# Attention in a gated MLP kernel: where the probabilities are divided by their sums

## The reference, cut to what matters

```python
k_sum = k.reshape(B, H, nb, block, D).max(axis=3)
v_sum = v.reshape(B, H, nb, block, D).mean(axis=3)
scores_l = scale * np.matmul(q, k.transpose(0, 1, 3, 2))
mask_l = np.abs(pos[:, None] - pos[None, :]) < window
scores_s = scale * np.einsum('bhsd,bhnd->bhsn', q, k_sum) + np.log(block)
scores_all = np.concatenate([np.where(mask_l, scores_l, -1e9), scores_s], axis=-1)
a = np.exp(scores_all - np.max(scores_all, axis=-1, keepdims=True))
a = a / (np.sum(a, axis=-1, keepdims=True) + 1e-09)
attn_out = np.matmul(a, np.concatenate([v, v_sum], axis=2))
```

## Time and profile before

| | us |
|---|---|
| median of 3 runs | 357.35 |
| lowest and highest | 356.35 and 358.55 |
| span of the profiled execution | 357.2 |
| VectorE busy in the span | 233.7 |
| TensorE busy in the span | 320.7 |
| ScalarE and GpSimd busy in the span | 150.7 and 136.4 |

### The profile page before, as it was taken

One profiled execution on the slowest core, in us unless ns is written; L12 is line 12 of the kernel. 1 busy time (PEld: TensorE's weight loads), 2 busy tenths in 40 slices (PEclk: granted clock), 3 DMA queues, 4 the chain that ended last, 5 costly groups with the idle time before them and its releaser, 6 DMA issues.

```text
span 357.2 us, 5495 instructions
## 1 busy us (share of the span) xinstructions
PE 320.7 (90%) x1876; PEld 292.6 (82%) x1876; DVE 233.7 (65%) x638; ACT 150.7 (42%) x416; POOL 136.4 (38%) x118
## 2 busy tenths in 40 slices
PE   8777967775778899996999999999999999999997
PEld 7666856765668788985799999988889999998886
DVE  6799999999999999979888200028886633331000
ACT  3375656664677676363322322243333211112222
POOL 5219367339434212599205700004444933331000
PEclk9899899999999999999899999999999999999999
DMA  8896774266331221233100000011211000001222
GB/s 180 143 212 146 164 167 108 62 157 143 91 87 50 57 67 59 73 119 89 46 0 1 2 0 2 0 44 46 73 30 31 29 2 0 0 2 59 88 109 98
DMA packets 49721, 25.33 MB, mean 71 GB/s; under 512 B 44170, under 2 KB 44446, under 8 KB 49310
## 3 DMA queue, kind: packets, MB, share of 16 engines
q1 hardware_dynamic: 49694, 24.99, 27.7%
HBM read 21.24 MB, written 3.15 MB: 68 GB/s over the span
## 4 chain that ended last, share of the span: by engine, by line
PE 56%; DVE 23%; issue 10%; POOL 5%; DMA 3%; SPq 1%; ACT 1%; DVEq 0%; POOLq 0%
PE psum L592 52%; DVE probs L858 6%; DVE neg_s L839 6%; DVE gate L901 3%; POOL g_lo L458 2%; DMA v_blk<-in_v_dram 2%; DVE sums_eps L847 2%; POOL win_v_lo L458 2%; DVE k_max L871 1%; DVE recip L852 1%; PE psum L675 1%; DVE k_a L880 1%; POOL win_u_lo L458 1%; PE psum L544 1%; DMA raw<-in_moe_w_in_dram 1%
## 5 line engine op out<-in xcount | busy, mean ns | idle before, releaser
L858 DVE TENSOR_SCALAR probs<-probs,recip 128x184 f32<-128x184 f32 x96 | 60.9, 675 | 1.7
L718 ACT ACTIVATE probs<-neg_s,neg_max 128x184 f32<-128x184 f32 x96 | 42.2, 441 | 44.8 <-DVE neg_max L839 44.5
L458 POOL TENSOR_TENSOR g_lo<-work,g_hi 128x384 fp32r<-128x384 f32 x32 | 36.3, 1147 | 46.8 <-ACT g_hi L819 25.8
L544 PE MATMUL psum<-ident,probs 128*128 128x128 f32 x144 | 25.8, 288 | 22.4 <-DVE probs L858 22.1
L901 DVE SCALAR_TENSOR_TENSOR gate<-xT,conv_c,gate 128x384 f32<-128x384 f32 (+8 forms) x44 | 41.7, 956 | 1.3
L544 PEld LDWEIGHTS psum<-ident,probs 128*128 128x128 f32 x144 | 16.0, 143 | 29.4 <-DVE probs L858 28.7
L458 POOL TENSOR_TENSOR vn_lo<-work,vn_hi 128x512 fp32r<-128x512 f32 x12 | 15.5, 1293 | 57.2 <-DVE vn_hi L1040 57.2
L839 DVE CUSTOM_DVE_ANT_0 neg_s<-psum,mask 128x184 f32<-128x184 f32 x96 | 29.2, 340 | 0.0
L1018 DVE TENSOR_TENSOR wsp_lo<-psum,wsp_hi 128x384 fp32r<-128x384 f32 x12 | 6.6, 548 | 33.6 <-ACT wsp_hi L800 33.6
L458 POOL TENSOR_TENSOR x_lo<-xT,x_hi 128x768 fp32r<-128x768 f32 x8 | 15.0, 1869 | 32.2 <-DVE x_hi L863 32.2
L1050 DVE TENSOR_TENSOR work<-psum,b_row 128x384 f32<-128x384 f32 x16 | 8.9, 558 | 27.8 <-PE psum L592 26.2
(11 more groups left out here) (125 smaller groups left out, 791.3 us busy)
## 6 DMA issues: line engine op xcount, KB each, us to landing
k_nat<-in_k_dram SPq DMA_DIRECT2D x16, 192.0 KB, 3.2
q_nat<-in_q_dram SPq DMA_DIRECT2D x16, 192.0 KB, 3.3
v_blk<-in_v_dram SPq DMA_DIRECT2D x4, 768.0 KB, 7.6
out_dram<-work SPq DMA_DIRECT2D x11, 256.0 KB, 2.0
v_main<-in_v_dram SPq DMA_DIRECT2D x16, 160.0 KB
raw<-in_moe_w_spatial_dram SPq DMA_DIRECT2D x6, 384.0 KB, 3.0
raw<-in_moe_w_out_dram SPq DMA_DIRECT2D x8, 256.0 KB, 2.7
raw<-in_moe_w_in_dram SPq DMA_DIRECT2D x8, 256.0 KB, 2.9
```

Source lines behind the costliest of these rows:

```text
L458: nc.gpsimd.tensor_tensor(dst_lo, src, dst_hi.bitcast(F32), ALU.subtract).then_inc(lo_sem, 1)
L544: ins = nc.tensor.transpose(bank_t(i)[:, n * P:(n + 1) * P], probs[:, i % 4, c:c + P], ident[:, :])
L718: ins = nc.scalar.activation(probs[:, i % 4, w], neg_s[:, i % 3, w], ACT.Exp, bias=neg_max[:, i % 4, h:h + 1], scale=-1.0, accum_out=sums[ ...
L858: ins = nc.vector.tensor_scalar(a, a, recip[:, i % 4, h:h + 1], None, ALU.mult)
```

## The change

The probabilities go into the products undivided. `invert_sums` writes the reciprocal of each of the two sums of a row 64 times, into a tile of 128x128 instead of 128x2. A TensorE transpose with the identity (`spread_recip`) lays this tile over the rows of the transposed output: row d of head h holds, at column q, the reciprocal of the sum of query q in head h. It goes into the two free quarters of the bank that holds the output of the same steps. ScalarE copies the undivided output to `xT` as before, but waits for the transposes, and a new VectorE instruction, `scale_x`, multiplies `xT` in place with the spread reciprocals from PSUM, for two steps at once. `high_x` and the taps wait for `scale_x`. On VectorE `normalise` goes, `scale_x` stands at the start of every odd step, and the loop has four steps more; the last halves of taps and the last two `split_wout` are placed anew in them. The exponentials wait for `add_eps` of four steps before.

```diff
--- before.py
+++ after.py
@@ -120,7 +120,7 @@
                 neg_max = sb("neg_max", [P, 4, 2], F32, att)
                 sums = sb("sums", [P, 4, 2], F32, att)
                 sums_eps = sb("sums_eps", [P, 4, 2], F32, att)
-                recip = sb("recip", [P, 4, 2], F32, att)
+                recip = sb("recip", [P, 4, P], F32, att)
                 probs = sb("probs", [P, 4, SC], F32, att)
                 probsT = sb("probsT", [P, 2, 3 * P], F32, att)
             win_v_hi = sb("win_v_hi", [P, C, DM], F32R, early)
@@ -164,7 +164,8 @@
         exp_done = sem("exp_done")
         eps_added = sem("eps_added")
         recip_ready = sem("recip_ready")
-        probs_ready = sem("probs_ready")
+        spread_done = sem("spread_done")
+        x_taken = sem("x_taken")
         probs_turned = sem("probs_turned")
         probsT_ready = sem("probsT_ready")
         x_summed = sem("x_summed")
@@ -537,7 +538,7 @@
                                  stop=True).then_inc(scores_ready, 1)
 
             def turn_probs(i):
-                pe.wait_ge(probs_ready, i + 1)
+                pe.wait_ge(exp_done, i + 1)
                 if i >= 2:
                     pe.wait_ge(probsT_ready, i - 1)
                 for n, c in enumerate((MAIN_A, MAIN_B, REST)):
@@ -560,6 +561,12 @@
                 nc.tensor.matmul(o, v_main[:, s, t, D:D + P], pT[:, P:2 * P], start=False, stop=False)
                 nc.tensor.matmul(o, v_rest[:, s, t, :], pT[:, 2 * P:3 * P], start=False,
                                  stop=True).then_inc(x_summed, 1)
+
+            def spread_recip(i):
+
+                pe.wait_ge(recip_ready, i + 1)
+                n = 2 * P + i % 2 * P
+                nc.tensor.transpose(bank_x(i)[:, n:n + P], recip[:, i % 4, :], ident[:, :]).then_inc(spread_done, 1)
 
             def turn_wout(c):
                 wait_piece(pe, W_OUT + c)
@@ -645,6 +652,7 @@
                     turn_probs(i - 3)
                 if 4 <= i:
                     values(i - 4)
+                    spread_recip(i - 4)
 
             for kind, n in groups[2:place["u", 0]]:
                 if kind == "val":
@@ -713,6 +721,7 @@
                 act.wait_ge(masked, i + 1)
                 if i >= 4:
                     act.wait_ge(probs_turned, i - 3)
+                    act.wait_ge(eps_added, i - 3)
                 for h in range(2):
                     w = slice(h * HEAD, (h + 1) * HEAD)
                     ins = nc.scalar.activation(probs[:, i % 4, w], neg_s[:, i % 3, w], ACT.Exp,
@@ -733,10 +742,10 @@
 
             def take_x(j):
 
-                act.wait_ge(x_summed, 2 * j + 2)
+                act.wait_ge(spread_done, 2 * j + 2)
                 p, r = divmod(2 * j, T)
                 nc.scalar.activation(xT[:, p, r * P:(r + 2) * P], bank_x(2 * j)[:, 0:2 * P],
-                                     ACT.Copy).then_inc(xT_ready, 1)
+                                     ACT.Copy).then_inc(x_taken, 1)
 
             def turned_wout(c):
                 act.wait_ge(wout_turned, c + 1)
@@ -849,14 +858,18 @@
 
             def invert_sums(i):
                 dve.wait_ge(eps_added, i + 1)
-                nc.vector.reciprocal(recip[:, i % 4, :], sums_eps[:, i % 4, :]).then_inc(recip_ready, 1)
-
-            def normalise(i):
-                dve.wait_ge(recip_ready, i + 1)
-                for h in range(2):
-                    a = probs[:, i % 4, h * HEAD:(h + 1) * HEAD]
-                    ins = nc.vector.tensor_scalar(a, a, recip[:, i % 4, h:h + 1], None, ALU.mult)
-                ins.then_inc(probs_ready, 1)
+                if i >= 4:
+                    dve.wait_ge(spread_done, i - 3)
+                nc.vector.reciprocal(recip[:, i % 4, :].rearrange("p (h d) -> p h d", d=D),
+                                     sums_eps[:, i % 4, :].rearrange("p (h d) -> p h d", d=1).broadcast_to(
+                                         (P, 2, D))).then_inc(recip_ready, 1)
+
+            def scale_x(j):
+
+                dve.wait_ge(x_taken, j + 1)
+                p, r = divmod(2 * j, T)
+                x = xT[:, p, r * P:(r + 2) * P]
+                nc.vector.tensor_tensor(x, x, bank_x(2 * j)[:, 2 * P:4 * P], ALU.mult).then_inc(xT_ready, 1)
 
             def high_x(p):
                 dve.wait_ge(xT_ready, T // 2 * (p + 1))
@@ -945,10 +958,10 @@
                 conv(tap // TAPS, tap % TAPS, (half,))
                 halves_done += 1
 
-            for i in range(STEPS + 2):
+            for i in range(STEPS + 6):
                 p, t = divmod(i, T)
-                if i >= 2:
-                    normalise(i - 2)
+                if i >= 7 and i % 2 == 1:
+                    scale_x((i - 7) // 2)
                 if i == 0:
                     add_blocks(0)
                 if i == 1:
@@ -962,7 +975,7 @@
                     mask_scores(i, 1)
                 if 0 <= i - 1 < STEPS:
                     add_eps(i - 1)
-                if t == 5 and p >= 1:
+                if t == 5 and 1 <= p < PAIRS:
                     high_x(p - 1)
                 if i < STEPS and p >= 2 and (t in (0, 1, 4) or p == PAIRS - 1):
                     conv_half()
@@ -975,11 +988,11 @@
                     split_wout(i - 2 - (PAIRS - 1) * T)
                 if 0 <= i - 1 < STEPS:
                     invert_sums(i - 1)
-                if i >= STEPS:
-                    for _ in range(3):
+                if i in (STEPS + 1, STEPS + 2):
+                    split_wout(i - STEPS + 1)
+                if STEPS <= i < STEPS + 4:
+                    for _ in range(2):
                         conv_half()
-            split_wout(2)
-            split_wout(3)
             while halves_done < 2 * TAPS * ATT_GATES:
                 conv_half()
             high_x(PAIRS - 1)
```

## The result

The changed kernel takes 359.44 us, the median of 20 runs (358.1 to 362.53), against 357.46 of the kernel before (20 runs, 355.57 to 359.85): a ratio of 1.0063, 95% interval 1.0039 to 1.0087. It is 0.6% slower, some 2 us, where 12 us were forecast. The profiled execution has a span of 357.4 us, only 0.2 more than before.

The account below looks back on a forecast made before the run. VectorE was taken to bound attention: work -30.7 + 45.6 + 8.4 = +23.3 us, held time -11.5, waits +2, with some 1.5 hidden, made +12: 369 us. Its own range was 362 to 374, the full range 345 to 377.

Parts of the forecast that it names:

- Part 1: VectorE in attention: two normalisations and the old reciprocal leave 48 steps, 30.7 us less work, held time not counted.
- Part 2: VectorE in attention: the widened reciprocal at 7 ns per element, 0.95 us in each of 48 steps, 45.6 us added.
- R1: Rival, chance 0.30: the reciprocal is short (0.28 us) and a loop through ScalarE's copy and scale_x sets attention, 348 us.
- Part 3: VectorE in attention: scale_x every other step, 24 x 0.35 us, 8.4 us added, not held by GpSimd.
- Part 4: TensorE in attention: 48 transposes, 6.7 us, cost nothing unless VectorE came down to some 106 us.
- Part 5: VectorE in attention: scale_x waits for ScalarE's copy, nearly covered by VectorE's other work; 2 us added in all.
- Part 6: VectorE held by GpSimd in attention: 8.4 us less at x_lo, net zero at k_a and k_b, 11.5 us less in all.
- the first pair: Start of attention: some 1.5 us hidden behind the loads, so 14 us longer attention makes the step +12.
- The break-even: Reciprocal on VectorE: forecast and no change part at 0.70 us from start to start, 5.0 ns per element.
- R2: Rival, chance 0.14: costs cancel, by a reciprocal of 4 to 6 ns per element or 22 us less held time; 358 us.

Follow-up runs that it names:

- a_short: Changed kernel with a two-element reciprocal and a maximum over single elements that spreads it: 348.11 us, ratio 0.9697 to the kernel before.
- a_both_late: Changed kernel with a two-element reciprocal spread by a maximum, no addition of 1e-9, and scale_x behind the mask: 336.42 us, ratio 0.9404.
- b_wide: Kernel before with the reciprocal widened to 128x128 and the normalisations kept: 384.13 us, ratio 1.0738.
- b_unheld: Kernel before with the two normalisations in a form that also sums its output: 356.02 us, ratio 0.994.
- a_epsacc: Changed kernel with the addition of 1e-9 in a form that also sums its output: 345.97 us, ratio 0.9662 to the kernel before.
- a_best: Changed kernel with a two-element reciprocal spread by a maximum, the 1e-9 addition in the summing form, and scale_x behind the mask: 338.5 us, ratio 0.9477.
- b_best: Kernel before with the normalisations and the addition of 1e-9 both in the summing form: 344.42 us, ratio 0.9627.
- b_unheld_noeps: Kernel before with the normalisations in the summing form and the addition of 1e-9 left out: 342.12 us, ratio 0.9564.

## Why the prediction was wrong

It named the bound and both kinds of cost, but its sum came out 10 us too high, because most of its terms were each off to the same side. The step that failed is the size of the work added, parts 2 and 3, +23.3 us forecast and some +16 found; the largest single term is the reciprocal's price. Then come the held time, 3 us short, and the wait.

- *Part 1, removed work*: 30.7 us forecast, 31.1 found (22.1 of normalisations and 9.0 of old reciprocals with the idle time behind them, all 48 steps).
- *Part 2, the reciprocal*: the term that was mis-sized. 7 ns per element forecast, (943 - 156) / 126 = 6.2 found; 0.86 us from start to start for 0.95, 41.3 us for 45.6. The prediction's estimate from the Trainium skill, page "VectorE: DVE Perf Modes", section "Walkthrough: the 8-slice pipeline in each mode", 8.3 ns with eight cycles taken for the repeat count of 8, is too much, and the 2 ns between the medians far too little; the measurement decides. `a_short` shows that this price is what separates the change from R1.
- *Part 3 and the masks*: 7 us for 8.4, and 1.5 us less for the masks, which wasn't foreseen. With parts 1 and 2 the work is some +16, not +23.3.
- *Part 4, the transpose*: nothing, as forecast, in the change. In `a_both_late` TensorE comes near the 106 us that the part named for the stage (101.5 of 110 us).
- *Part 5, the wait*: 2 us forecast, 0.5 found, since the long reciprocal covers it. With the short one it is 7.6 and 11.1 us; that its cover is then gone, the part had said.
- *Part 6, the held time*: 11.5 us less forecast, some 15 found. Around the pair shown, `x_lo` holds `sums_eps` for 0.5 us (forecast 0.4, though 1.81 + 0.16 - 1.49 is 0.48), `k_a` and `k_b` hold for 1.0 + 1.3 (forecast 3.0). The 30.6 us held at L858 that the prediction starts from is too low: 60.9 is the time in which at least one of these overlapping instructions ran, and 96 durations of 675 ns are 64.8, so 34.5 were held. The 11.5 doesn't hang on it, as it was added up event by event.
- *The sum*: the first pair was to hide 1.5 us, and nothing in the account asks for it. Some +16 of work, -15 of held time and 0.5 of new idle time make +1 to +2, where the forecast had 12.
- *What it started from*: it took the profiled execution, 357.2 us, for the timed median of 357.35. By the 1.7 to 1.8 us between a run's time and its span it was a slower execution, near 359.0. That shifts no term of the sum.
- *The break-even* of 5.0 ns per element hung on the other terms: with those found it is 6.2 less 2.3 / (48 x 0.126), some 5.9. The real price was just above it.

So the time came near R2's 358 us, which had a chance of 0.14. R2 had two ways there, a reciprocal of 4 to 6 ns, or 22 us less held time because long reciprocals that are never held lie beside GpSimd's work. What happened lies between them, 6.2 ns and 15 us, and the cause that R2 gave for the second is shown in `b_wide` (11 us) but not in the change, where `a_short` has as little held time with a short reciprocal. So R2's number came near without its mechanism, and that work and held time cancel almost to the microsecond is luck. The range from 345 to 377 held the time; the forecast's own, 362 to 374, did not.

What stays open: how much held time comes back at other instructions. In `b_unheld` 8 to 12 us were expected back and 21 came, in `a_epsacc` 5 were expected and 3 came, and no rule that would have given both was found.

## What to carry to other kernels

Before work is moved off the bound engine, ask which of its time is work and which is being held, and by what form of instruction: held time goes to the next instruction of that kind, so removing one carrier gives back only what has no successor, and changing the form of the last carriers is the cheap cure (14 us off the changed kernel here for one more output of a two-element instruction). An instruction whose cost per element the trace shows only at one or two elements is the first thing to price, before it is widened; widened 64 times it takes 41 us of work here, more than the two products over 184 columns that the change removed (22 us). The cure isn't free for a wide instruction: the summing form takes 402 ns over 184 columns where the plain one takes 316.

## What was not expected of the hardware

- The reciprocal on VectorE takes 6.2 ns per element (943 ns at 128, 156 at 2); a maximum over single elements writes a 128x128 tile in 286 ns.
- `tensor_scalar` with an accumulator output was never held beside GpSimd (at most 155 ns for two elements, in 144 instructions of `a_epsacc`, `a_best` and `b_best`, and 408 for 184, in 288 of `b_unheld`, `b_unheld_noeps` and `b_best`), while the plain form was held for up to 2 us (2269 ns at most). The Trainium skill, page "SBUF — State Buffer", section "Who interferes with whom", lists the form as an exception among those that can take both ports, and these runs agree.
- A tap with two SBUF inputs is held like the plain form: 1.95 us instead of 0.61 behind `k_b`. So is the cast `x_hi`: 2.40 us instead of 0.55 in `a_epsacc`.
